# Second feed-forward layer of a sliding-window attention kernel: chunks of 4x512 and 256 tokens become six of 384

## What is computed

```
scores = scale * q @ k.T, masked to 0 <= i - j < 64
attn   = softmax(scores) @ v            -> x, 2304 tokens x 512
h = x @ w_in   ; g = max(0.01 h, h)     ; x = g @ w_out      (layer 1, 512 -> 2048 -> 512)
h = x @ w_in2  ; g = h * cos(h)         ; out = g @ w_out2   (layer 2, same sizes)
```

## Time and profile before

| | us |
|---|---|
| median of 3 runs (899.45 to 900.46) | 900.28 |
| the profiled execution | 900.46 |
| its span, first to last instruction | 897.7 |
| TensorE busy | 871.0 |
| DVE busy | 418.1 |
| ACT busy | 369.6 |

### The profile page before, as it was taken

One profiled execution on the slowest core, in us unless ns is written; L12 is line 12 of the kernel. 1 busy time (PEld: TensorE's weight loads), 2 busy tenths in 40 slices (PEclk: granted clock), 3 DMA queues, 4 the chain that ended last, 5 costly groups with the idle time before them and its releaser, 6 DMA issues.

```text
span 897.7 us, 13153 instructions
## 1 busy us (share of the span) xinstructions
PE 871.0 (97%) x5040; PEld 719.9 (80%) x5040; DVE 418.1 (47%) x751; ACT 369.6 (41%) x849; POOL 90.3 (10%) x72
## 2 busy tenths in 40 slices
PE   5889999999999999999999899999999999999998
PEld 4778877787778877788888688888888888888897
DVE  4466444435443444443223454454455445544554
ACT  5566434334334343433444433343334333433443
POOL 3565000000000000001444300000000000000000
PEclk9999999999999999999999999999999999999999
DMA  6466202111112111004332400020002000200010
GB/s 207 153 193 218 75 26 75 63 37 61 50 63 75 35 63 50 13 1 142 101 100 84 139 1 0 0 93 0 0 0 93 0 0 0 72 1 1 1 48 23
DMA packets 29838, 52.90 MB, mean 59 GB/s; under 512 B 2528, under 2 KB 5984, under 8 KB 29792
## 3 DMA queue, kind: packets, MB, share of 16 engines
q1 hardware_dynamic: 29792, 52.24, 18.1%
HBM read 42.80 MB, written 9.44 MB: 58 GB/s over the span
## 4 chain that ended last, share of the span: by engine, by line
PE 90%; ACT 4%; DVE 3%; issue 2%; DMA 0%; POOL 0%; SPq 0%; DVEq 0%; ACTq 0%
PE h_ps L348 42%; PE y_ps L373 21%; PE y_ps L367 21%; PE st_ps L299 2%; PE st_ps L282 2%; PE st_ps L288 1%; ACT probs L444 1%; ACT w_hi L432 1%; DVE probs L590 1%; DVE neg_max L597 1%; ACT probsT L452 1%; DMA qk_sb<-qk 0%; DVE g_raw L643 0%; ACT g_hi L490 0%; DVE g_lo L665 0%
## 5 line engine op out<-in xcount | busy, mean ns | idle before, releaser
L348 PE MATMUL h_ps<-x_hi,w_hi 128*128 128x512 f32 (+1 forms) x640 | 242.2, 378 | 4.8 <-DVE g_raw L659 3.0
L348 PE MATMUL h_ps<-x_lo,w_hi 128*128 128x512 f32 (+1 forms) x640 | 237.4, 371 | 0.0
L348 PE MATMUL h_ps<-x_hi,w_lo 128*128 128x512 f32 (+1 forms) x640 | 237.3, 371 | 0.0
L348 PEld LDWEIGHTS h_ps<-x_hi,w_hi 128*128 128x128 f32 x640 | 122.0, 191 | 28.9 <-DVE g_raw L659 3.4
L665 DVE TENSOR_TENSOR g_lo<-g_raw,g_hi 128x512 fp32r<-128x512 f32 (+1 forms) x160 | 105.1, 657 | 85.8 <-ACT g_hi L490 85.8
L348 PEld LDWEIGHTS h_ps<-x_lo,w_hi 128*128 128x128 f32 x640 | 122.0, 191 | 20.6
L348 PEld LDWEIGHTS h_ps<-x_hi,w_lo 128*128 128x128 f32 x640 | 122.0, 191 | 19.6
L490 ACT ACTIVATE g_hi<-g_raw 128x512 fp32r<-128x512 f32 (+1 forms) x160 | 94.2, 589 | 104.6 <-DVE g_raw L643 52.6
L643 DVE TENSOR_TENSOR g_raw<-h_ps,act_in 128x512 f32<-128x512 f32 (+1 forms) x80 | 51.0, 637 | 175.0 <-ACT act_in L469 175.0
L256 POOL TENSOR_TENSOR w_lo<-w_raw,w_hi 128x512 fp32r<-128x512 f32 x64 | 86.1, 1367 | 409.6 <-ACT w_hi L432 409.4
L367 PE MATMUL y_ps<-g_hi,w_hi 128*128 128x512 f32 (+1 forms) x320 | 121.2, 379 | 0.1
(11 more groups left out here) (53 smaller groups left out, 789.4 us busy)
## 6 DMA issues: line engine op xcount, KB each, us to landing
qk_sb<-qk SPq DMA_DIRECT2D x36, 288.0 KB, 3.1
v_sb<-values SPq DMA_DIRECT2D x36, 256.0 KB, 2.8
w_raw<-w_in SPq DMA_DIRECT2D x32, 256.0 KB, 2.7
w_raw<-w_out SPq DMA_DIRECT2D x32, 256.0 KB, 2.8
layer_out<-y_out SPq DMA_DIRECT2D x4, 1024.0 KB, 5.8
x_raw<-layer_out SPq DMA_DIRECT2D x4, 1024.0 KB, 7.5
out<-y_out SPq DMA_DIRECT2D x4, 1024.0 KB, 5.0
mask_sb<-mask SPq DMA_DIRECT2D x4, 256.0 KB, 3.0
```

Source lines behind the costliest of these rows:

```text
L348: mm = pe.matmul(h_ps[:, j % 2, 0:width], w[:, j, cols], x[:, kt, 0:width], start=kt == 0 and a == 0, stop=kt == KT - 1 and a == 2)
```

## The change

Layer 2 gets a chunk width of its own, CH2 = 384, and so N2 = 6 equal chunks; layer 1 keeps its five. Up blocks of layer 2 are 12 matmuls of width 384, down blocks are 9 matmuls of width 512 (3 groups of 128 tokens). All the element-wise steps of layer 2 work on 384 columns, and a load of x is 768 KB. DVE copies one bank instead of two at each end of a layer-2 chunk, ACT still two. The last chunk has three output banks: ACT copies 0 and 2, DVE copies 1, and SP stores each by itself. The loops run N1 to LAST-1 (five chunks), and only the last chunk is written out. `turns` keeps its place in `probs`, and the output in DRAM is addressed by chunk. The diff, cut to its core (the same substitution of CH2 for the width in `sine`, `angle` and `times_cosine`, and the same loop in ACT's and DVE's programs, are left out):

```diff
 N1 = 1 + (TOK - FIRST) // WIDE
-N2 = N1
+CH2 = 384
+QT2 = CH2 // P
+N2 = TOK // CH2
 LAST = N1 + N2 - 1
...
         def width_of(n, layer):
-            return FIRST if isinstance(n, int) and n == (0 if layer == 1 else LAST) else WIDE
+            return CH2 if layer == 2 else FIRST if is_first(n) else WIDE
 
...
             def load_x(n):
-                start, width = WIDE * (n - N1), width_of(n, 2)
-                stored = 1 + next(c for c in range(N1) if sum(tokens(c)) >= start + width)
+                start = CH2 * (n - N1)
+                stored = 1 + next(c for c in range(N1) if sum(tokens(c)) >= start + CH2)
                 sp.wait_ge(x_ready, KT * n)
                 sp.wait_ge(y_stored, 16 * stored)
-                sp.dma_start(x_raw[:, :, 0:width], hidden_dram[:, :, start:start + width]).then_inc(x_in, 16)
+                sp.dma_start(x_raw[:, :, 0:CH2], hidden_dram[:, :, start:start + CH2]).then_inc(x_in, 16)
 
...
                 else:
-                    t = WIDE * (n - N1) // P
-                    y = y_out[:].rearrange("p (m d) -> p m d", d=DM)
-                    sp.dma_start(out[:, t:t + WIDE // P, :], y).then_inc(y_stored, 16)
+                    y = y_out[:, 0:QT2 * DM].rearrange("p (m d) -> p m d", d=DM)
+                    sp.dma_start(out[n - N1], y).then_inc(y_stored, 16)
 
...
             store_y(LAST - 1)
-            for m in range(2):
-                sp.wait_ge((y_act_done, y_dve_done)[m], LAST + 1)
-                sp.dma_start(out[:, NT - 2 + m, :], y_out[:, DM * m:DM * m + DM]).then_inc(y_stored, 16)
-            sp.wait_ge(y_stored, 16 * (LAST + 2))
+            for m in range(QT2):
+                if m == 1:
+                    sp.wait_ge(y_dve_done, LAST + 1)
+                else:
+                    sp.wait_ge(y_act_done, LAST + 1 + m // 2)
+                sp.dma_start(out[N2 - 1][:, m, :], y_out[:, DM * m:DM * m + DM]).then_inc(y_stored, 16)
+            sp.wait_ge(y_stored, 16 * (LAST + QT2))
 
...
                                        start=j == 0 and a == 0, stop=j == FT - 1 and a == 2)
-                    end = m == width_of(n, 2) // P - 1
+                    end = m == QT2 - 1
                 if final:
                     mm.then_inc(last_banks_done, 1)
                 elif end:
                     mm.then_inc(down_done, 1)
 
             def chunk(n, layer, attends, last=False, next_layer=None):
-                parts = 2 if last else KT
+                parts = KT if layer == 1 else QT2
                 for j in range(FT):
...
             chunk(N1 - 1, 1, False, next_layer=2)
-            with nc.Fori(N1, LAST - 1, engines=(pe.engine,), hint_back_edge=True) as n:
+            with nc.Fori(N1, LAST, engines=(pe.engine,), hint_back_edge=True) as n:
                 chunk(n, 2, False)
-            chunk(LAST - 1, 2, False)
             chunk(LAST, 2, False, last=True)
...
             def turns_in(n, j):
-                width = width_of(n, 2)
                 act.wait_ge(up_done, FT * n + j + 1)
-                act.activation(act_in[:, j % 2, 0:width], h_ps[:, j % 2, 0:width], ACT.Identity, scale=INV_2PI,
+                act.activation(act_in[:, j % 2, 0:CH2], h_ps[:, j % 2, 0:CH2], ACT.Identity, scale=INV_2PI,
                                bias=0.25).then_inc(act_in_done, 1)
 
             def sine(n, j):
-                width = width_of(n, 2)
                 act.wait_ge(angle_done, FT * n + j - L2 + 1)
-                act.activation(act_in[:, j % 2, 0:width], act_in[:, j % 2, 0:width], ACT.Sin,
+                act.activation(act_in[:, j % 2, 0:CH2], act_in[:, j % 2, 0:CH2], ACT.Sin,
                                scale=TWO_PI).then_inc(sine_done, 1)
...
                 act.wait_ge(y_stored, 16 * LAST)
-                act.wait_ge(last_banks_done, 1)
-                act.activation(y_out[:, 0:DM], y_ps[0][:, 0, :], ACT.Copy).then_inc(y_act_done, 1)
+                for m in (0, 2):
+                    act.wait_ge(last_banks_done, m + 1)
+                    act.activation(y_out[:, DM * m:DM * m + DM], y_ps[m // 2][:, 0, :],
+                                   ACT.Copy).then_inc(y_act_done, 1)
 
...
                             for kt in range(KT):
-                                split_x_block(kt, width_of(n + 1, 1 if attends else 2))
+                                split_x_block(kt, WIDE if attends else CH2)
                         if s == KT + 1:
...
                     dve.wait_ge(y_stored, 16 * n)
-                for m in range(2, KT):
+                for m in range(2, KT if layer == 1 else QT2):
                     last = dve.tensor_copy(y_out[:, width * m:width * m + width], y_ps[1][:, m - 2, 0:width])
...
     out = nc.dram_tensor("out", (TOK, DM), F32, kind="ExternalOutput").ap()
-    build(nc, *args, out.rearrange("(t p) d -> p t d", p=P))
+    build(nc, *args, out.rearrange("(c m p) d -> c p m d", m=QT2, p=P))
     r = run_bass_kernel_spmd(nc, [arrays], core_ids=[0])
```

More of the change, by code:

```diff
@@ L102, in build @@
         row_inv = sb("row_inv", [P, PRING, 4])
-        turns = probs[:, 0, :]
+        turns = probs[:].rearrange("p a b -> p (a b)")[:, 0:CH2]
         def two_banks(name):
@@ L573, in _ @@
             split_weights(2 * FT - 1)
-            with nc.Fori(N1, LAST - 1, engines=(act.engine,), hint_back_edge=True) as n:
+            with nc.Fori(N1, LAST, engines=(act.engine,), hint_back_edge=True) as n:
                 chunk(n, 2, False)
-            chunk(LAST - 1, 2, False)
             chunk(LAST, 2, False, last=True)
@@ L647, in angle @@
                 tile = FT * n + j
-                width = width_of(n, 2)
                 dve.wait_ge(act_in_done, tile + 1)
-                dve.tensor_scalar(turns[:, 0:width], act_in[:, j % 2, 0:width], ROUND, ROUND, ALU.add,
+                dve.tensor_scalar(turns, act_in[:, j % 2, 0:CH2], ROUND, ROUND, ALU.add,
                                   ALU.subtract).then_inc(turns_done, 1)
                 dve.wait_ge(turns_done, tile - L2 + 1)
-                dve.tensor_tensor(act_in[:, j % 2, 0:width], act_in[:, j % 2, 0:width], turns[:, 0:width],
+                dve.tensor_tensor(act_in[:, j % 2, 0:CH2], act_in[:, j % 2, 0:CH2], turns,
                                   ALU.subtract).then_inc(angle_done, 1)
             def times_cosine(n, j):
-                width = width_of(n, 2)
                 dve.wait_ge(sine_done, FT * n + j - L2 + 1)
-                dve.tensor_tensor(g_raw[:, j % 2, 0:width], h_ps[:, j % 2, 0:width], act_in[:, j % 2, 0:width],
+                dve.tensor_tensor(g_raw[:, j % 2, 0:CH2], h_ps[:, j % 2, 0:CH2], act_in[:, j % 2, 0:CH2],
                                   ALU.mult).then_inc(g_raw_done, 1)
@@ L701, in chunk @@
                             for kt in range(KT):
-                                split_x_block(n + 1, kt, width_of(n + 1, 1 if attends else 2))
+                                split_x_block(n + 1, kt, WIDE if attends else CH2)
                         if s == KT + 2:
@@ L727, in _ @@
             chunk(N1 - 1, 1, False)
-            with nc.Fori(N1, LAST - 1, engines=(dve.engine,), hint_back_edge=True) as n:
+            with nc.Fori(N1, LAST, engines=(dve.engine,), hint_back_edge=True) as n:
                 chunk(n, 2, False)
-            chunk(LAST - 1, 2, False)
             chunk(LAST, 2, False, last=True)
```

## The result

Six chunks of 384 take 909.17 us (median of 4 runs, 908.70 to 911.93) against 899.87 before: 1.011 times, 95% interval 1.0095 to 1.0125. That is 9.3 us slower, where 3.0 were forecast. The profiled execution took 909.83 us, 9.4 more than the one before; its span is 908.0, 10.3 more. The difference lies outside the instructions, 1.8 us here and 2.8 before. What follows accounts for the span.

A forecast was written before the change was run, and what follows sets the result against it. TensorE, busy 871.0 of 897.7 us, was taken as the bound. Terms +2.3 - 0.24 - 0.5 + 1.5 = +3.0 us gave 903.3 us against the median 900.28; range 898.5 to 905.5, likeliest case 902.0 to 905.0.

The forecast's parts named there:

- part 1: Pace of layer 2's matmul blocks on TensorE: +2.3 us in sum, between -1.6 and +12.
- lose nothing of this kind: Down blocks beside narrower up blocks: the old last chunk's small loss was assumed gone at width 384, -0.3 us.
- 192 more matmuls at 13.3 ns: Layer 2's up blocks: 1152 matmuls of width 384 at 173.3 ns, 199.7 us in all, 2.6 us more.
- Rival 1: Up blocks: pace proportional to width, 170.0 ns at 384; 3.9 us less, 899.4 us, no change; chance 0.18.
- part 3: Where layer 2 begins: longer TensorE waits for the first down and third up blocks, +1.5 us in sum.
- part 2: Layer 2's element-wise chain keeps up with TensorE at zero cost; chunk ends save 0.24 us, the last tile 0.5.
- the chunk ends: Ends within layer 2: no wait for bank copies, removing the wait at the old last chunk's start, -0.24 us.
- the last tile's wait: TensorE's wait at the last tile falls from 0.66 us to 0.08 plus restart 0.08, -0.5 us.
- The third up block's wait: Start of layer 2: TensorE's wait for DVE would be 4.1 us instead of 3.2, +1.0 us.
- Rival 2: Start of layer 2: DVE's 7.41 us loop-entry gap doesn't come back; 6.1 us below forecast, 897.2 us; chance 0.12.
- rival 4: DVE's two extra loop back edges each stall like its loop entry, 5.8 us each, 915 us; chance 0.03, shared with slower pace.
- Rival 3: Start of layer 2: the clock doesn't fall after the wait; 1.9 us less, 901.4 us, no change; chance 0.04.

The follow-up runs named there:

- width-384 run: The changed kernel with layer 2's down matmuls moving only 384 of the 512 output features; 860.38 us, one run.
- held-back runs: Layer 1's last store and the x load behind it held until DVE is in its layer-2 loop: kernel before 895.50 us, changed kernel 906.31.
- nine downs: The kernel before with 9 of the 12 down matmuls per tile in layer 2's 512-token chunks; 857.88 us, one run.
- width 448: The changed kernel with layer 2's down matmuls moving 448 of the 512 output features; 886.44 us, one run.
- two and two: The changed kernel with TensorE's layer-2 order made two up blocks, then two down blocks; 910.44 us, one run.

## Why the prediction was wrong

The direction was right, and the size was off: 3.0 us forecast, 9.3 measured, above the range.

- **The step that failed is in part 1**: "I assume that 384 is wide enough to lose nothing of this kind, -0.3; were it 0.02 a tile as there, it would be 96 x 0.02 = +1.9." The loss with 384 beside 512 is 0.067 us a tile. Some 90 tiles have both changes (at each chunk end two blocks of a kind follow each other): 6.0 us for a term set at zero, and three times the +1.9 that was allowed for it. The sign was on the rows: the earlier trace rows had 1.39 us for 6 x 226.7 ns = 1.36 beside narrow up blocks. I took the loss of the 256-wide chunk as an upper bound for 384, though nothing said that it falls with the difference; no experiment gives a rule for it either.
- The rest of part 1 held: 192 more matmuls at 13.3 ns, 2.6 us, shown by the flat 173.3 ns of the width-384 run. Rival 1 (170.0) fell. Part 1 in all: 10.3 of span, less 3.0 of part 3, plus 0.8 of part 2, leaves 8.1; the pieces give 2.6 + 6.0 - 0.3 = 8.3. (The stretch of the earlier trace rows has three ends of chunks in it and not two; nothing hangs on it.)
- Part 2 held: the chain kept up, the chunk ends lost nothing, and the last tile's wait went: -0.24 and -0.58 against -0.24 and -0.5.
- Part 3 was 3.0 instead of 1.5. The first down block lost 0.7 more than before instead of 0.5. The third up block's wait was 4.45 and not 4.1, because the gap did not shrink with the smaller load: 7.41 again. That the bulk lengthens the gap is shown by the held-back runs; that it does so by holding up DVE's instructions is read from the packet on queue 14. The 0.6 us that a smaller load was to save did not come; the store and the load were issued 0.2 us later against the gap's start (1.0 us ahead of it instead of 1.2), which hides a part of it at most. The clock fell for 6.8 us instead of 3.4, 1.1 us more. The length of the wait does not decide it: after waits of 4.6 us (nine downs) and 4.9 (width 448) it fell for 3.4, after 4.2 (two and two) and 5.4 (width 384) for 6.8. What does is left open.
- Rival 2 (the gap goes away) and rival 4 (each back edge stalls) did not happen: entries at the four back edges took 0.2 us. Rival 3 went the other way.

That the loss is in TensorE and needs no other engine is argued, from its repeating within 1 ns in every tile; what in TensorE makes it is open.

## What to carry to other kernels

Where two kinds of matmul alternate on a TensorE that is never idle, keep their moving widths equal, or measure the mixed pair: a pace taken from blocks of one width does not hold for the mixture, and a few hundredths of a us in a block is many us in the sum. Count each narrower chunk at a fixed price per extra matmul, 13.3 ns here at 256, 384 and 512, and measure any other width: 448 had 20.0. And look at what an engine's first pass into a loop meets: DVE stood there for 7.4 us with 2 MB of traffic beside it, and writing that pass out, or issuing the traffic a few us later, won 4.5 to 5 us in the kernel before.

## What the hardware showed that I had not expected

- Float32r matmuls at full clock: 120.0, 173.3, 206.7 and 226.7 ns at width 256, 384, 448 and 512. At the half clock 320 and 427 ns at 384 and 512, which is width / 1.2 with no fixed part.
- The change from 512 to 384 costs 0.026 us, over the first six matmuls, and the change from 384 to 512 0.041, over nine. Between 384 and 448 there is no such loss, and none at equal widths, but for the 0.027 us at the five first up blocks of a chunk.
- With quiet DMA queues DVE still stood 3.3 us at its loop entry; an 8 KB packet on queue 14 came 1.6 us into it.
- DVE's `angle` steps took 1.11 and 1.68 us beside GpSimd's f32 subtraction, 0.43 and 0.69 alone.
